# Convolution blocks as 98 rows of 64 columns instead of 49 rows of 128

## The reference

```python
h_filt = (np.maximum(pos_emb @ w1, 0.0) @ w2) * np.exp(-0.01 * pos)[:, None]
u = x * v
Uf = np.fft.rfft(u, n=2 * S, axis=1)
Hf = np.fft.rfft(h_filt, n=2 * S, axis=0)
y = np.fft.irfft(Uf * Hf[None], n=2 * S, axis=1)[:, :S, :]
x = x * y
h = x @ moe_w_in;  x = np.maximum(h, 0.0) ** 2 @ moe_w_out
h = x @ moe2_w_in; return (np.maximum(h, 0.0) + alpha * np.minimum(h, 0.0)) @ moe2_w_out
```

## Time and profile before

| | us |
|---|---|
| median of 3 runs (range) | 1552.01 (1550.06 to 1558.69) |
| the profiled execution | 1558.79 |
| its span | 1556.7 |
| PE busy in the span | 1527.4 (98%) |
| DVE / ACT / POOL busy | 970.6 / 719.9 / 68.9 |

### The profile page before, as it was taken

One profiled execution on the slowest core, in us unless ns is written; L12 is line 12 of the kernel. 1 busy time (PEld: TensorE's weight loads), 2 busy tenths in 40 slices (PEclk: granted clock), 3 DMA queues, 4 the chain that ended last, 5 costly groups with the idle time before them and its releaser, 6 DMA issues.

```text
span 1556.7 us, 19100 instructions
## 1 busy us (share of the span) xinstructions
PE 1527.4 (98%) x7302; PEld 1331.2 (86%) x7302; DVE 970.6 (62%) x1118; ACT 719.9 (46%) x864; POOL 68.9 (4%) x51
## 2 busy tenths in 40 slices
PE   8989999997999999999999999999999999999998
PEld 8878888886988888888888888888888888888887
DVE  4336666662556666666666666666666666666664
ACT  1222333330345545545555555555555555555553
POOL 1520000112010000000000000000000000000000
PEclk9999999996899999999999999999999999999999
DMA  4744565635310011100000000000000000000000
GB/s 156 216 121 128 163 214 166 209 107 157 87 43 17 28 27 28 28 21 14 7 8 0 6 6 6 6 6 6 6 6 6 6 6 0 6 6 6 6 7 13
DMA packets 37506, 80.18 MB, mean 52 GB/s; under 512 B 3692, under 2 KB 20016, under 8 KB 35120
## 3 DMA queue, kind: packets, MB, share of 16 engines
q1 hardware_dynamic: 35296, 69.51, 14.5%
q10 hardware_dynamic: 2160, 9.97, 2.0%
HBM read 60.24 MB, written 19.23 MB: 51 GB/s over the span
## 4 chain that ended last, share of the span: by engine, by line
PE 96%; DMA 3%; DVE 0%; POOL 0%; issue 0%; ACT 0%; SPq 0%; ACTq 0%
PE ps L169 12%; PE ps L171 12%; PE ps L158 12%; PE ps L159 12%; PE ps L170 12%; PE ps L160 12%; PE ps L603 4%; PE ps L533 3%; PE ps L542 1%; PE ps L568 1%; PE ps L559 1%; PE ps L551 1%; PE ps L543 1%; PE ps L552 1%; PE ps L560 1%; PE ps L553 1%
## 5 line engine op out<-in xcount | busy, mean ns | idle before, releaser
L327 DVE SCALAR_TENSOR_TENSOR g<-ps,relu 128x960 f32<-128x960 f32 x208 | 240.8, 1158 | 207.5 <-ACT relu L275 204.6
L275 ACT ACTIVATE relu<-ps 128x960 f32<-128x960 f32 x208 | 202.6, 974 | 309.9 <-PE ps L160 309.9
L352 DVE TENSOR_TENSOR g_lo<-g,g_hi 128x960 fp32r<-128x960 f32 x208 | 240.7, 1157 | 168.0 <-ACT g_hi L288 168.0
L169 PE MATMUL ps<-g_hi,w_hi 128*128 128x480 f32 x832 | 320.9, 386 | 1.0 <-DVE g_lo L361 1.0
L171 PE MATMUL ps<-g_lo,w_hi 128*128 128x480 f32 x832 | 319.4, 384 | 0.0
L159 PE MATMUL ps<-x_hi,w_lo 128*128 128x480 f32 x832 | 317.0, 381 | 0.0
L158 PE MATMUL ps<-x_hi,w_hi 128*128 128x480 f32 x832 | 316.6, 381 | 0.1
L170 PE MATMUL ps<-g_hi,w_lo 128*128 128x480 f32 x832 | 316.6, 381 | 0.0
L288 ACT CAST g_hi<-g 128x960 fp32r<-128x960 f32 x208 | 207.0, 995 | 232.6 <-DVE g L327 232.6
L160 PE MATMUL ps<-x_lo,w_hi 128*128 128x480 f32 x832 | 313.8, 377 | 0.0
L361 DVE SCALAR_TENSOR_TENSOR g_lo<-ps,g_hi 128x960 fp32r<-128x960 f32 x208 | 239.4, 1151 | 12.8 <-ACT g_hi L295 12.8
(11 more groups left out here) (74 smaller groups left out, 1201.4 us busy)
## 6 DMA issues: line engine op xcount, KB each, us to landing
work<-dft SPq DMA_DIRECT2D x49, 384.0 KB, 3.4
g_dram<-work SPq DMA_DIRECT2D x49, 256.0 KB, 2.2
gt<-g_dram SPq DMA_DIRECT2D x16, 784.0 KB
x<-x_gate ACTq DMA_DIRECT2D x4, 1560.0 KB, 6.9
out_t<-x SPq DMA_DIRECT2D x26, 240.0 KB, 2.0
gt<-x_seq SPq DMA_DIRECT2D x22, 196.0 KB
gt<-v_seq SPq DMA_DIRECT2D x22, 196.0 KB
a_u<-pos_t SPq DMA_DIRECT2D x8, 392.0 KB, 6.9
```

Of the source, the lines that this page charges most:

```text
L169: nc.tensor.matmul(acc[layer][:, :T], w_hi[k][:, at], hi[:, c], start=first, stop=False)
L275: nc.scalar.activation(relu1[:], h[0][:, :, :T], ACT.Relu).then_inc(relu1_ready, 1)
L327: nc.vector.scalar_tensor_tensor(out=g1[:], in0=h[0][:, :, :T], scalar=0.0, in1=relu1[:], op0=ALU.max, op1=ALU.mult).then_inc(g1_ready, 1)
L352: nc.vector.tensor_tensor(g_lo[0][:, s // 2 % 2], g1[:], g_hi[0][:, s // 2 % 2].bitcast(FP32), ALU.subtract).then_inc(g1_lo_ready, 1)
```

## The change

NB = 2 blocks of R = 98 rows by N1 = 64 columns. The row transform now gives 98 complex frequencies; each has a column transform of length 64. Real and imaginary parts lie on the two halves of the partitions (`HALF`), so that one complex transform of length 64 is one real matmul with a 128x128 matrix. A step k handles the two frequencies 2k and 2k + 1; there are still 49 steps. `dft128` has three 128x128 matrices for each frequency (before: six for each step), 384 KB a step as before.

- Stage 1: each chunk is moved out by both engines, ScalarE its first block and VectorE its second, in two instructions each over 64 partitions (one for the real, one for the imaginary half; some write other partitions than they read). For the filter's 16 chunks VectorE's part is four `tensor_tensor` that add or subtract ScalarE's output (`add_shifted_block`); the row table no longer has this.
- Stage 2: `unit_spectra` is 2 matmuls of 128 columns, `u_spectra` 2, `filter_spectra` 2 and `inverse` 4 of 256 columns. `filter_copy` writes the filter's spectrum and a second copy with its halves exchanged, in three instructions, to `filt`, now in `gt`'s memory. `spectra_products` multiplies with both copies; `inverse` sums the two products by matmuls.
- Stage 3: GN = 4 columns a group, two accumulating matmuls of 98 columns for each; still 8 matmuls a half and 32 halves. `load_group` reads two runs of 4 KB for a partition instead of one of 8 KB.

```diff
-N1, N2, R = P, 49, 98
+NB, N1, R = 2, 64, 98
+K_STEPS = R // 2
...
-GN = 8
+GN = 4
 GROUPS = N1 // GN
...
         wait(sp, last_done, 2 * (q - 1))
-        sp.dma_start(gt[:R, q % 2], g_dram[:, GN * q:GN * (q + 1), :]).then_inc(gt_loaded[q % 2], 16)
+        sp.dma_start(gt[:R, q % 2], g_halves[:, :, GN * q:GN * (q + 1), :]).then_inc(gt_loaded[q % 2], 16)
...
-            sp.dma_start(g_dram[2 * k:2 * k + 2].rearrange("r n w -> n r w"), g_sb[:, k % 3]
+            sp.dma_start(g_dram[4 * k:4 * k + 4].rearrange("(k r) n w -> (r n) k w", r=2), g_sb[:, k % 3]
                          ).then_inc(g_stored[k % 3], 16)
...
             if n >= 4:
-                pe.wait_ge(copied_dve if n % 2 else copied_act, (n - 4) // 2 + 1)
+                pe.wait_ge(copied_0, n - 3)
+                pe.wait_ge(copied_1, n - 3)
...
             for c in range(CH):
                 data = slots[j % SLOTS][:, 0, c, :] if j >= 0 else h_sb[:, CH * n + c, :]
                 last = nc.tensor.matmul(two_banks(n % 4)[:, 256 * c:256 * c + 2 * R], data,
-                                        dft98_sb[:, int(j < 0), :], start=True, stop=True)
+                                        dft98_sb[:], start=True, stop=True)
...
         def unit_spectra(k):
             pe.wait_ge(mats_loaded[k % LOADS], 16 * (k // LOADS + 1))
             wait(pe, r_hat_copied, k - 1)
-            out, m = ps[:, 2 + k % 2, :2 * P], mats[:, k % LOADS]
-            sin_cos, cos_neg = (m[:, n:n + 2].rearrange("p m k -> p (m k)") for n in (0, 1))
-            nc.tensor.matmul(out, a_r_rows[:, k, 1], sin_cos, start=True, stop=False)
-            nc.tensor.matmul(out, a_r_rows[:, k, 0], cos_neg, start=False, stop=True).then_inc(r_hat_done, 1)
+            for i in range(2):
+                last = nc.tensor.matmul(ps[:, 2 + k % 2, P * i:P * (i + 1)], a_r_rows[:, 2 * k + i],
+                                        mats[:, k % LOADS, i, :P], start=True, stop=True)
+            last.then_inc(r_hat_done, 1)
 
         def u_spectra(k):
             wait(pe, u_used, k - 1)
-            out, m = ps[:, k % 2, :], mats[:, k % LOADS]
-            sin, cos, neg = m[:, 0], m[:, 1], m[:, 2]
-            re, im = a_u_rows[:, k, 0], a_u_rows[:, k, 1]
-            nc.tensor.matmul(out[:, :256], cos, re, start=True, stop=False)
-            nc.tensor.matmul(out[:, :256], sin, im, start=False, stop=True)
-            nc.tensor.matmul(out[:, 256:], cos, im, start=True, stop=False)
-            nc.tensor.matmul(out[:, 256:], neg, re, start=False, stop=True).then_inc(u_done, 1)
+            for i in range(2):
+                last = nc.tensor.matmul(ps[:, k % 2, 256 * i:256 * (i + 1)], mats[:, k % LOADS, i, :P],
+                                        a_u_rows[:, 2 * k + i], start=True, stop=True)
+            last.then_inc(u_done, 1)
 
         def filter_spectra(k):
             pe.wait_ge(r_hat_copied, k + 1)
             wait(pe, filt_copied, k - 1)
-            out = ps[:, 4 + k % 2, :]
-            nc.tensor.matmul(out[:, :256], r_hat[:, k % 2, 0], w2_sb, start=True, stop=True)
-            nc.tensor.matmul(out[:, 256:], r_hat[:, k % 2, 1], w2_sb, start=True, stop=True).then_inc(filt_done, 1)
+            for i in range(2):
+                last = nc.tensor.matmul(ps[:, 4 + k % 2, 256 * i:256 * (i + 1)], r_hat[:, k % 2, i], w2_sb,
+                                        start=True, stop=True)
+            last.then_inc(filt_done, 1)
 
         def inverse(k):
             pe.wait_ge(y_ready, k + 1)
             wait(pe, g_copied, k - 1)
-            out, m = ps[:, 6 + k % 2, :], mats[:, k % LOADS]
-            sin, cos, neg = m[:, 3], m[:, 4], m[:, 5]
-            re, im = (ys[:, k % 3, i].rearrange("p b c -> p (b c)") for i in range(2))
-            nc.tensor.matmul(out[:, :256], cos, re, start=True, stop=False)
-            nc.tensor.matmul(out[:, :256], neg, im, start=False, stop=True)
-            nc.tensor.matmul(out[:, 256:], cos, im, start=True, stop=False)
-            nc.tensor.matmul(out[:, 256:], sin, re, start=False, stop=True).then_inc(inv_done, 1)
+            for i in range(2):
+                out, at = ps[:, 6 + k % 2, 256 * i:256 * (i + 1)], slice(256 * i, 256 * (i + 1))
+                for n in range(2):
+                    last = nc.tensor.matmul(out, mats[:, k % LOADS, i, P * (n + 1):P * (n + 2)],
+                                            products[:, k % 3, n, at], start=n == 0, stop=n == 1)
+            last.then_inc(inv_done, 1)
 
...
         for n in range(GN):
-            last = nc.tensor.matmul(ps[:, 6 + blk, 64 * n:64 * (n + 1)], gt[:R, q % 2, n, blk * P:(blk + 1) * P],
-                                    idft98_sb[:R], start=True, stop=True)
+            for half in range(2):
+                last = nc.tensor.matmul(ps[:, 6 + blk, R * n:R * (n + 1)],
+                                        gt[:R, q % 2, half, n, blk * P:(blk + 1) * P], idft98_sb[:R, half],
+                                        start=half == 0, stop=half == 1)
         last.then_inc(last_done, 1)
...
-    def copy_stage1(copy, n, copied):
-        src = two_banks(n % 4).rearrange("p (c w) -> p c w", w=256)[:, :, :2 * R]
+    def stage1_part(n, blk, part):
+
+        src = two_banks(n % 4).rearrange("p (c w) -> p c w", w=256)[HALF[blk], :, R * part:R * (part + 1)]
         j = n - R_CHUNKS
-        dst = a_u_out[:, :, :, CH * j:CH * (j + 1)] if j >= 0 else a_r_out[:, :, :, CH * n:CH * (n + 1)]
-        copy(dst, src.rearrange("p c (s k) -> p k s c", s=2)).then_inc(copied, 1)
+        out, at = (a_u_out, CH * j) if j >= 0 else (a_r_out, CH * n)
+        return src.rearrange("p c k -> p k c"), out[HALF[part], :, blk, at:at + CH]
...
         def filter_copy(k):
             act.wait_ge(filt_done, k + 1)
             wait(act, u_used, k - 1)
-            nc.scalar.copy(filt[:, k % 2].rearrange("p b c -> p (b c)"), ps[:, 4 + k % 2, :]).then_inc(filt_copied, 1)
+            nc.scalar.copy(filt[:, k % 2, 0], ps[:, 4 + k % 2, :])
+            for part in range(2):
+                last = nc.scalar.copy(filt[HALF[part], k % 2, 1], ps[HALF[1 - part], 4 + k % 2, :])
+            last.then_inc(filt_copied, 1)
...
-        for n in range(0, R_CHUNKS + U_CHUNKS, 2):
+        for n in range(R_CHUNKS + U_CHUNKS):
             act.wait_ge(spec_done, n + 1)
-            copy_stage1(nc.scalar.copy, n, copied_act)
+            for part in range(2):
+                src, dst = stage1_part(n, 0, part)
+                last = nc.scalar.copy(dst, src)
+            last.then_inc(copied_0, 1)
...
-        def products(k):
+        def spectra_products(k):
             dve.wait_ge(u_done, k + 1)
             dve.wait_ge(filt_copied, k + 1)
-            u = ps[:, k % 2, :].rearrange("p (r b c) -> p r b c", r=2, b=2)
-            f = filt[:, k % 2]
-            nc.vector.tensor_tensor(u0h, u[:, :, 0:1, :].to_broadcast([P, 2, 4, P]),
-                                    f.unsqueeze(1).to_broadcast([P, 2, 4, P]), ALU.mult)
-            f0 = f.rearrange("p (r b) c -> p r b c", b=2)[:, :, 0, :]
-            nc.vector.tensor_tensor(u1h, u[:, :, 1:2, :].to_broadcast([P, 2, 2, P]),
-                                    f0.unsqueeze(1).to_broadcast([P, 2, 2, P]), ALU.mult).then_inc(u_used, 1)
+            wait(dve, inv_done, k - 2)
+            u = ps[:, k % 2, :].rearrange("p (k b c) -> p k b c", k=2, b=NB)
+            f = filt[:, k % 2].rearrange("p v (k b c) -> p v k b c", k=2, b=NB)
+            y = products[:, k % 3].rearrange("p v (k b c) -> p v k b c", k=2, b=NB)
+            for v in range(2):
+                nc.vector.tensor_tensor(y[:, v], u[:, :, 0:1, :].to_broadcast([P, 2, NB, P]), f[:, v], ALU.mult)
+            nc.vector.tensor_tensor(cross[:, k % 2], u[:, :, 1, :].unsqueeze(1).to_broadcast([P, 2, 2, P]), f[:, :, :, 0, :],
+                                    ALU.mult).then_inc(u_used, 1)
             dve.wait_ge(u_used, k + 1)
-            wait(dve, inv_done, k - 2)
-            y = ys[:, k % 3]
-            nc.vector.tensor_tensor(y[:, 0], u0h[:, 0, 0:2], u0h[:, 1, 2:4], ALU.subtract)
-            nc.vector.tensor_tensor(y[:, 1], u0h[:, 0, 2:4], u0h[:, 1, 0:2], ALU.add)
-            nc.vector.tensor_tensor(z[:, 0], u1h[:, 0, 0], u1h[:, 1, 1], ALU.subtract)
-            nc.vector.tensor_tensor(z[:, 1], u1h[:, 0, 1], u1h[:, 1, 0], ALU.add).then_inc(add_done, 1)
-            dve.wait_ge(add_done, k + 1)
-            nc.vector.tensor_tensor(y[:, :, 1, :], y[:, :, 1, :], z, ALU.add).then_inc(y_ready, 1)
+            nc.vector.tensor_tensor(y[:, :, :, 1, :], y[:, :, :, 1, :], cross[:, k % 2], ALU.add).then_inc(y_ready, 1)
+
+        def add_shifted_block(n):
+            for part in range(2):
+                src, dst = stage1_part(n, 1, part)
+                other = a_r_out[HALF[1 - part], :, 0, CH * n:CH * (n + 1)]
+                for odd in range(2):
+                    at = slice(odd, R, 2)
+                    last = nc.vector.tensor_tensor(dst[:, at], src[:, at], other[:, at],
```

(58 more changed lines are left out.)

72 lines of the change are left out of this document (32 added, 40 removed).

## The result

| | before | after |
|---|---|---|
| median, us (range, 4 runs each) | 1551.03 (1548.88 to 1558.69) | 1500.72 (1499.05 to 1503.86) |
| the profiled execution / its span, us | 1558.79 / 1556.7 | 1503.86 / 1501.8 |
| stage 2, us | 257.0 | 209.8 |
| from the end of stage 2 to the end, us | 1199.2 | 1193.9 |

The ratio is 0.967, with a 95% interval of 0.964 to 0.970: 50.3 us less, where 52.5 were forecast (1499.5). Between the two profiled executions the difference is 54.9 us.

What follows compares the result with a forecast made beforehand. TensorE was taken to bound stage 2 and nearly all of stage 3. Terms -63.2 - 0.7 + 1 + 5.2 + 1.0 + 4 + 0.2 = -52.5 us, on a median of 1552.0, gave 1499.5 us; range 1488 to 1514.

Steps and rivals of the forecast that it cites:

- -63.2 us for TensorE's columns: Stage 2: fewer matmul columns shorten TensorE's step from 5.18 to 3.89 us, over 49 steps; -63.2 us.
- ScalarE's +1 us for ordinary steps: Stage 2: ScalarE's chain of copies makes the next `filter_spectra` at most 0.1 us late; 1 us charged for all steps.
- +5.2 us for twelve pieces: Stage 2: in 12 steps a piece of weights ahead of `unit_copy` makes TensorE 0.43 us late; +5.2 us.
- The seven DMA issues on ScalarE, put at nothing: Stage 2: ScalarE's seven DMA issues run beside the copy ahead of them; no cost.
- +4 us for the tables: Stage 2: table loads have 6.6 us of lead instead of 9.2, some land late; +4 us, bounds 0 and 12.
- rival B: Stage 2: the DMA, full beside the weights' loads, holds it; +8 to +10 us, 1509 us; chance 0.12.
- +1.0 and -0.7 us for start and end of stage 2: Start: ScalarE's copies delay `filter_spectra(2)` about 1.3 us, +1.0 us net; end: VectorE's chain 2.74 for 3.47 us, -0.7 us.
- Stage 1, +0.2 us: Filter's chunks stay at 1.33 us each; the copy behind the last becomes two instructions, +0.2 us; bounds -0.2 and 10.
- Stage 3, 0 us: Matmuls of 98 columns cost 0.216 us, as those of 64 and 128 do; no change.
- rival C: Stage 3: matmuls are paid by column, 0.331 us each; +29 us, 1529 us; chance 0.04.
- Rivals D and E: Stage 2: D, partition-crossing half copies cost a multiple, 1582 us, chance 0.03; E, `unit_spectra`'s 128-column matmuls cost 0.432, 1520 us, 0.02.

Runs made afterwards that it cites:

- e3: Kernel after, with the two 128-column matmuls of `unit_spectra` issued twice in each step of stage 2; median 1512.64 us, ratio 0.974 to the kernel before.
- e4: Kernel after without ScalarE's second, exchanged copy of the filter's spectrum (products read the first copy twice, results wrong); median 1495.97 us, ratio 0.963.
- e1: Kernel after, but ScalarE rounds each piece of weights ahead of `filter_copy` instead of behind `result_copy`; median 1500.69 us, ratio 0.967.
- the repeat: The kernel after, unchanged, run and profiled a second time; median 1501.25 us, ratio 0.967 to the kernel before.
- e2: Kernel after, but SyncE issues each table's load ahead of the store of the result instead of behind it; median 1492.95 us, ratio 0.964.
- before again: The kernel before, unchanged, profiled a second time; 1556.22 us in one run.
- e7: Kernel after with 64 instead of 98 columns in stage 3's 256 matmuls, leaving out part of the result; median 1506.80 us, ratio 0.971.
- filling: Kernel after with early pieces and early table loads, plus 24 useless matmuls ahead of the `gt` waits of stage 3's halves 0 and 2; median 1490.62 us, ratio 0.960.

## Why the prediction was right, point by point

**-63.2 us for TensorE's columns** held: 3.90 us a step for 3.89, in every kernel that keeps stage 2's matmuls, and 4.35 with two matmuls more (`e3`). This term is nearly the whole result, and it came from two pitches of starts, not from durations.

**ScalarE's +1 us for ordinary steps**: nothing is late there; `e4` shows no gain from a shorter chain. I had let the copies overlap at every pair; three of four don't, so `result_copy` starts at 2.86 us behind `filter_spectra` instead of 2.79. That used part of the reserve in ordinary steps.

**+5.2 us for twelve pieces** is 12 x 0.50 = 6.0, the same 0.07 us each. `e1` shows the mechanism by taking it away.

**The seven DMA issues on ScalarE, put at nothing**, cost 0.45 us: six are hidden, but that of `w_out` lasts 0.87 us and makes its step 4.35. Why it lasts longer no run varied.

**+4 us for the tables** is 6.4 in the first profile and 1.9 in the repeat; both lie within the bounds of 0 and 12. The term's base was the lateness of one load. Left out was what a wait can do to the clock: the longest wait of 1.85 us cost 3.8, so about 2 of the 6.4 us are the clock's. By `e2` the cause is that loads are issued behind the store; rival B named the place rightly and the DMA's rate wrongly.

**+1.0 and -0.7 us for start and end of stage 2**: the two stand at 5.9 us against 3.2 before, 2.7 more, where 0.3 were forecast and 1 us more for all steps. The wait of `filter_spectra(2)` for ScalarE is 1.88 us for 1.3, since its six copies follow each other at 0.60 us and not at 0.48. Most of the miss, 1.7 us, is again the clock, which fell behind this wait. VectorE's last chain is shorter as forecast. Together with pieces and tables stage 2 came to 209.8 us for 204.3, and to 205.4 in the repeat.

**Stage 1, +0.2 us**: the 16 chunks take 21.32 us, the number of before. Stage 2 began at 98.09 us after 100.46 before; this is spread of the executions, since the kernels with the same stages 0 and 1 began it from 96.17 to 103.75, and before again at 101.22.

**Stage 3, 0 us**, is the step that failed. The price of a matmul was right (1.76 us a half for 1.73, 1 us for all 32; rival C, +29 us, falls). The table of costs in the Trainium skill, "VectorE: DVE Perf Modes", section on the TRN2 errata, by which the prediction had estimated 14.5 us, doesn't agree either; the measurement decides. But I took the price at the full clock and asked nothing about the 45 us in which the clock was at 0.54. Behind stage 2 the kernel gained 5.3 us. `e7`, which changes only the columns, takes the gain away.

So in the first profile 5.5 us too little were charged in stage 2, and about as much was missed as a gain in stage 3. That the two cancel is luck: 1500.7 for 1499.5 is closer than the working deserves. In the repeat stage 2 is only 1.1 us over its forecast. Rivals D and E fall with the 581 ns of a half copy and the 3.90 us of a step.

Still open is why the clock comes back sooner in the kernels with 98 columns, though a matmul takes the same time. No run varied this alone beyond 64 and 98.

## What to carry to other kernels

Where an engine sets the step, count its starts at full pitch, and then price again every wait that had been hidden by the old, longer step: loads issued behind a store and work issued ahead of what the next step needs cost nothing at 5.18 us and up to 12 us at 3.90. Moving two lines each got 7.3 us back (1501.25 to 1493.99). And where the granted clock is low, look at it as a term of its own: an edit can move it without changing any price at the full clock, and a wait of 1.85 us can cost 3.8.

## What the runs showed of the hardware that was not expected

- The matmuls of 98 columns and of 64 take the same at each level of the clock (0.22 us at 2.4 GHz, 0.41 to 0.47 at 1.2). But in the nine profiles with 98 columns and no filling the full clock came back 27 to 31 us behind stage 2, and in the three with 64 columns 37 to 44 us behind it.
- At the start of stage 2 TensorE waited 1.88 us in the kernel after and 1.87 us in `e2_table_first`, in the same place of the same work; behind it the granted clock was 0.50 in the one and 1.00 in the other. Idles of 1.85 us (kernel after) and 2.10 us (`e1_pieces_early`) for a table were followed by 0.51 and 0.54, idles of 2.16 us (the same kernel) and 1.59 us (`e4_one_copy`) by 1.00. So the length of the one idle alone doesn't decide, and what does stays open.
- ScalarE's copies of 512 elements are followed by the next instruction after 0.48 to 0.49 us where partitions stay the same, and after 0.585 to 0.60 where they change; the busy time of one is 0.58 to 0.59 in both cases.
- SyncE's issue of a table's load lasted 0.33 us in every step when it stood ahead of the store, and 0.47 to 2.24 us right behind it (`e2_table_first` and the kernel after).
